# A linear-attention, soft-MoE and feed-forward kernel: the decay tables leave the start of attention, r is scaled out of PSUM, the state's decay goes to GpSimd, half of w1 is loaded in the last chunk

## The chip, the cores and the metric

The kernel runs on one core of a Trainium2 chip. The metric is the device time of one execution in microseconds (us), lower is better. Engines are called as the profile calls them: PE (TensorE; PEld is its weight loads), DVE (VectorE), ACT (ScalarE), POOL (GpSimd), SP (the queue that issues the DMAs here).

## What is computed

Three stages, in float32. First a linear attention with a decaying state, for 4 batches, 8 heads, 768 tokens, head size 48:

```
for t in range(S):
    y[:, :, t] = einsum('bhd,bhde->bhe', r_t, state + outer(u * k_t, v_t))
    state = w * state + outer(k_t, v_t)
```

Its output, 3072 tokens of 384 values, goes through a soft mixture of 8 experts with 4 slots each (logits x @ phi, softmax over tokens and over slots, two matrices w1 and w2 per expert), and then through a feed-forward layer with ELU (w_in 384x2048, w_out 2048x384).

## The kernel before, in words

Attention is done in chunks of 128 tokens: 6 chunks of 4 batches, which are 24 units (un = 4c + b). Inside a chunk the decay is folded into r and k: r is multiplied by powers of w that fall with the token's place, k by powers that grow, so that one matrix product gives all scores of the chunk. Each unit holds 8 heads as 4 pairs, head sizes padded from 48 to 64 (HP), so that a pair fills 128 partitions once it is turned.

**The tables.** DVE builds the powers transposed (head dimension on partitions, token along the row) from L841 to L858: seven squarings, then a doubling of the filled columns, each step waiting for the one ahead; they lie in the buffer of scores. PE turns them into PSUM (L505), DVE multiplies the first r and k out of PSUM (L866), ACT copies the tables to SBUF (L1120) for all later units.

**A unit.** POOL scales r into r_nat (L461), multiplies r by u and by k for the bonus of the diagonal (L466, L468), and scales k into k_nat (L479). PE turns r_nat (turn_r, L512) and k_nat (turn_k, L519); ACT copies the turned r to r_pair (L1100), DVE the turned k to k_pair (L879). PE multiplies the two into the scores in PSUM (attend, L530), adds the old state's part (state_in, L542), turns the former unit's output (turn_x, L569), and multiplies scores with v (values, L561) and k with v (key_values, L552). DVE reduces the bonus (L874), ACT writes the diagonals of the scores (L1106, 8 instructions a unit in two halves), DVE copies the masked scores over them (masked, L884, two a unit), keeps the state (L924 or L926, and the decay L936), and moves the turned output (L890). ACT takes the output out of PSUM (L1111). In each chunk's first two units PE and DVE also make the logits of the chunk ahead (L576, L582, L897 to L903).

**The order** is written out by hand and the same on every engine: in the body of unit un, PE does key_values(un), attend(un+1), state_in(un), turn_x(un-1), turn_r and turn_k(un+2), values(un). DVE does state_sum(un), bonus(un+2), masked(un+1, 0), the decay of un, x_to_sbuf(un-1), masked(un+1, 1), k_to_sbuf(un+2). ACT does y_to_sbuf(un-1), the diagonals of un+1, r_to_sbuf(un+2). The scores have one PSUM buffer, so attend(un+1) waits until both masked copies of un are done (L526). SP loads r and k four units ahead, v three units ahead, and one expert of w1 in every third unit (L351); w2, w_in and w_out follow when their space is free. Most of these last lie over buffers of attention.

After attention (its last values end at 130.8 us) come the expert layers and from about 178 us the feed-forward layer, in which PE is busy throughout.

Of the kernel before, what the change touches and what calls it, by code (L numbers as in the profile page):

```python
# [19 lines left out]
F32 = mybir.dt.float32  # L20
# [6 lines left out]
P = 128  # L27
# [9 lines left out]
def attention_moe_ffn_kernel(nc, r, k, v, w, u, phi, w1, w2, w_in, w_out, out):  # L37
# [22 lines left out]
    with ExitStack() as ctx:  # L60
# [27 lines left out]
        r_raw = place("r_raw", [P, B, H, D], F32)  # L88
        k_raw = place("k_raw", [P, B, H, D], F32)
        u_row = place("u_row", [P, H, D], F32)  # L90
        r_table = place("r_table", [P, H, D], F32)
        k_table = place("k_table", [P, H, D], F32)
        r_nat = place("r_nat", [P, 2, H, HP], F32)
        k_nat = place("k_nat", [P, 2, H, HP], F32)
        assert cursor[0] >= EARLY_AT + 2 * W2_BYTES
# [5 lines left out]
        SCORES_END = cursor[0]  # L101
        y_T = place("y_T", [P, PAIRS, B * P], F32)
        r_pair = place("r_pair", [P, 2, PAIRS, P], F32)
        k_pair = place("k_pair", [P, 2, PAIRS, P], F32)
# [93 lines left out]
        ps_warm = banks[7][:, 0:P]  # L198
# [21 lines left out]
        cleared = sem("cleared")  # L220
        ones_set = sem("ones_set")
        spread_ready = sem("spread_ready")
        powers = sem("powers")
        tables_T = sem("tables_T")
        tables_turned = sem("tables_turned")
        tables_ready = sem("tables_ready")

        r_scaled = sem("r_scaled")
# [80 lines left out]

        PE_TOP_T, PE_TOP_ROWS, PE_SLOT_IN, PE_DEN, PE_SLOT_T = range(1, 6)  # L310
# [23 lines left out]
        def _(sp):  # L334
            def load_rk(c, b):
                tokens = bass.ds(c * P, P)
                sp.dma_start(r_raw[:, b], r_dram[b, tokens]).then_inc(rk_loaded[b], 16)
                sp.dma_start(k_raw[:, b], k_dram[b, tokens]).then_inc(rk_loaded[b], 16)
# [88 lines left out]
        def _(pool):  # L427
# [3 lines left out]
            pool.memset(ones[:, :], 1.0).then_inc(ones_set, 1)  # L431
            pool.memset(ident[:, :], 0.0).then_inc(const_set, 1)
# [15 lines left out]
            pool.memset(r_nat[:, :, :, D:HP], 0.0).then_inc(cleared, 1)  # L448
            pool.memset(k_nat[:, :, :, D:HP], 0.0).then_inc(cleared, 1)
            pool.memset(state[:, :, :, D:HP], 0.0).then_inc(cleared, 1)  # L450
            pool.memset(x_sb[:, :, DM:XW], 1.0).then_inc(cleared, 1)

            def scale_chunk(c, first, last):
                for b in range(B):
                    un, i = c * B + b, b % 2
                    pool.wait_ge(rk_loaded[b], 32 * (c + 1))
                    wait_for(pool, r_turned, un - 1)
                    if first and b == 1:
                        pool.wait_ge(tables_ready, 1)
                    if not (first and b == 0):  # L460
                        pool.tensor_tensor(r_nat[:, i, :, 0:D], r_raw[:, b], r_table[:, :, :],  # L461
                                           ALU.mult).then_inc(r_scaled, 1)
                    pool.wait_ge(r_scaled, un + 1)
                    if first and b == 0:
                        pool.wait_ge(u_loaded, 16)
                    pool.tensor_tensor(r_raw[:, b], r_raw[:, b], u_row[:, :, :], ALU.mult).then_inc(ru_done, 1)  # L466
                    pool.wait_ge(ru_done, un + 1)
                    pool.tensor_tensor(r_raw[:, b], r_raw[:, b], k_raw[:, b], ALU.mult).then_inc(ruk_done, 1)  # L468
                    if first and b == 0:
                        continue  # L470
                    if first and b == 1:
                        pool.wait_ge(tables_ready, 2)
# [796 lines left out]
```

## Time and profile before

| | us |
|---|---|
| median of 3 runs (407.63 to 408.87) | 407.9 |
| the profiled execution, device time | 407.67 |
| its span, first to last instruction | 405.5 |
| PE busy | 384.7 (95%) |
| DVE busy | 275.8 (68%) |
| ACT busy | 219.3 (54%) |
| POOL busy | 114.7 (28%), of it nearly all in attention |
| DMA moved | 51.84 MB |

The profiled execution's own time lies 2.2 us above its span. The busy shares are means over three different stages, so they say little about attention: that has to be read from windows and from the order of time.

### The profile page before, as it was taken

What the parts mean: (1) busy time and instruction counts of PE and PEld (TensorE: products, weight loads), DVE (VectorE), ACT (ScalarE), POOL (GpSimd) and SP (SyncE); (2) the same over time, 40 slices, a digit from 0 to 9 for tenths busy, and PEclk for the clock granted to TensorE, in tenths of its full rate; (3) what the DMA queues carried; (4) which work ended last, traced back from release to release, by engine and by line L of the source; (5) the groups of instructions that cost most, each with busy time, mean ns of one, the idle gap of its engine ahead of it and who ended that gap; (6) DMA issues with size and microseconds to landing.
All of it is one profiled execution on the core that took longest, in us unless ns stands there. A gap on an engine that the chain in (4) does not pass through costs nothing.

```text
span 405.5 us, 9559 instructions
## 1 busy us (share of the span) xinstructions
PE 384.7 (95%) x3528; PEld 341.6 (84%) x3528; DVE 275.8 (68%) x527; ACT 219.3 (54%) x502; POOL 114.7 (28%) x131
## 2 busy tenths in 40 slices
PE   6689999999998799988999999999999999999997
PEld 5588888888886435357999999999999999999996
DVE  4687777877765661079987677677676676776771
ACT  2676757676775214076655544645645465446441
POOL 4998778787870000037410000000000000000000
PEclk8999999999999999999999999999999999999999
DMA  6989899899987879970002000200100020002002
GB/s 128 184 241 259 161 265 267 190 234 270 240 251 290 305 291 423 401 222 18 0 2 78 2 0 2 78 0 0 45 33 0 0 78 0 0 0 78 2 0 78
DMA packets 84802, 51.84 MB, mean 128 GB/s; under 512 B 76704, under 2 KB 81952, under 8 KB 82336
## 3 DMA queue, kind: packets, MB, share of 16 engines
q1 hardware_dynamic: 84768, 51.37, 43.0%
q8 instruction: 23, 0.38, 0.4%
q14 instruction: 11, 0.09, 0.1%
HBM read 45.86 MB, written 4.72 MB: 125 GB/s over the span
## 4 chain that ended last, share of the span: by engine, by line
PE 87%; DVE 5%; issue 3%; POOL 3%; ACT 2%; DMA 0%; SPq 0%; DVEq 0%; POOLq 0%; ACTq 0%
PE psum L823 16%; PE psum L824 16%; PE psum L825 16%; PE psum L530 6%; PE psum L740 5%; PE psum L561 5%; PE psum L569 3%; PE psum L542 3%; PE psum L682 3%; PE psum L663 3%; PE psum L512 2%; PE psum L519 2%; PE psum L552 2%; PE psum L576 2%; PE psum L644 1%
## 5 line engine op out<-in xcount | busy, mean ns | idle before, releaser
L823 PE MATMUL psum<-w_out_hi,elu_hi 128*128 128x384 f32 x372 | 124.8, 336 | 1.3 <-DVE elu_lo L1063 1.3
L824 PE MATMUL psum<-w_out_lo,elu_hi 128*128 128x384 f32 x372 | 125.0, 336 | 0.0
L825 PE MATMUL psum<-w_out_hi,elu_lo 128*128 128x384 f32 x372 | 124.3, 334 | 0.0
L1214 ACT ACTIVATE exp_h<-psum 128x512 f32<-128x512 f32 x95 | 57.1, 601 | 97.3 <-PE psum L740 97.3
L1075 DVE SCALAR_TENSOR_TENSOR elu<-psum,neg_part 128x512 f32<-128x512 f32 x95 | 65.6, 691 | 56.8 <-ACT neg_part L1201 56.8
L824 PEld LDWEIGHTS psum<-w_out_lo,elu_hi 128*128 128x128 f32 x372 | 69.8, 188 | 3.6
L823 PEld LDWEIGHTS psum<-w_out_hi,elu_hi 128*128 128x128 f32 x372 | 69.8, 188 | 2.1 <-DVE elu_lo L1063 2.1
L1063 DVE TENSOR_TENSOR elu_lo<-elu,elu_hi 128x512 fp32r<-128x512 f32 x95 | 69.9, 735 | 0.1
L825 PEld LDWEIGHTS psum<-w_out_hi,elu_lo 128*128 128x128 f32 x372 | 69.9, 188 | 0.0
L1106 ACT ACTIVATE scores<-ident,bonus 128x128 f32<-128x128 f32 x192 | 58.7, 391 | 1.1 <-DVE bonus L874 1.1
L1201 ACT ACTIVATE neg_part<-exp_h 128x512 f32<-128x512 f32 x95 | 59.2, 624 | 0.1
L884 DVE COPY_PREDICATED scores<-mask,psum 128x512 f32<-128x512 uint32 x48 | 35.3, 738 | 13.3 <-ACT scores L1106 11.7
L1088 DVE CAST elu_hi<-elu 128x512 fp32r<-128x512 f32 x95 | 41.5, 437 | 0.1
L740 PE MATMUL psum<-c_T,G_T 128*128 (+1 forms) x95 | 37.1, 392 | 0.1
L487 POOL TENSOR_TENSOR w_out_lo<-w_out_raw,w_out_hi 128x384 fp32r<-128x384 f32 x16 | 17.4, 1107 | 69.5 <-ACT w_out_hi L1183 69.5
L530 PE MATMUL psum<-r_pair,k_pair 64*128 64x128 f32 x384 | 27.9, 284 | 3.6 <-DVE k_pair L879 2.7
L530 PEld LDWEIGHTS psum<-r_pair,k_pair 64*128 64x128 f32 x384 | 23.6, 187 | 5.9 <-issue 3.9
L1111 ACT COPY y_T<-psum 128x512 f32<-128x512 f32 x24 | 14.0, 585 | 23.6 <-PE psum L561 23.6
L561 PE MATMUL psum<-scores,v_sb 128*64 128x128 f32 x384 | 26.3, 279 | 0.0
L466 POOL TENSOR_TENSOR r_raw<-r_raw,u_row 128x384 f32<-128x384 f32 x24 | 24.3, 1012 | 5.6 <-DVE r_nat L866 3.8
L479 POOL TENSOR_TENSOR k_nat<-k_raw,k_table 128x384 f32<-128x384 f32 x23 | 23.1, 1005 | 8.8 <-PE psum L552 8.8
L461 POOL TENSOR_TENSOR r_nat<-r_raw,r_table 128x384 f32<-128x384 f32 x23 | 23.2, 1010 | 5.1 <-DMA k_raw<-in_k_dram 5.1
(145 smaller groups left out, 428.3 us busy)
## 6 DMA issues: line engine op xcount, KB each, us to landing
w_sb<-in_moe_w_dram SPq DMA_DIRECT2D x8, 1536.0 KB, 7.9
w<-in_moe_w_dram SPq DMA_DIRECT2D x8, 1536.0 KB, 8.5
r_raw<-in_r_dram SPq DMA_DIRECT2D x24, 192.0 KB, 4.2
k_raw<-in_k_dram SPq DMA_DIRECT2D x24, 192.0 KB, 4.5
v_sb<-in_v_dram SPq DMA_DIRECT2D x24, 192.0 KB, 4.7
out_dram<-out_sb SPq DMA_DIRECT2D x24, 192.0 KB, 1.9
w_in_sb<-in_moe_w_in_dram SPq DMA_DIRECT2D x3, 1024.0 KB, 13.2
w_out_raw<-in_moe_w_out_dram SPq DMA_DIRECT2D x4, 768.0 KB, 12.2
```

What stands on the lines that cost most here:

```text
L530: m = pe.matmul(ps_A[two][:, a, :], k_pair[rows, i, a, :], r_pair[rows, i, a, :], start=True, stop=True)
L561: m = pe.matmul(ps_y[e0:e0 + HP, two, (a // 2) * P:(a // 2) * P + P], v_sb[:, b, h, :], scores[:, i, h, :], start=(first and a < 2), stop= ...
L740: pe.matmul(banks[4 + f % RING][:, :], G_T[:, f * P:(f + 1) * P], c_T[:, bass.ds(i * BANK, BANK)], start=True, stop=True).then_inc(ffn_don ...
L823: pe.matmul(acc, hi, w_out_hi[:, f, :], start=(f == 0), stop=False)
L824: pe.matmul(acc, hi, w_out_lo[:, f, :], start=False, stop=False)
L825: m = pe.matmul(acc, lo, w_out_hi[:, f, :], start=False, stop=(f == KF2 - 1))
L1063: dve.tensor_tensor(elu_lo[:, f % RING, :], elu[:, f % 2, :], elu_hi[:, f % RING, :].bitcast(F32), ALU.subtract).then_inc(lo_done, 1)
L1075: dve.scalar_tensor_tensor(out=elu[:, f % 2, :], in0=banks[4 + f % RING][:, :], scalar=0.0, in1=neg_part[:, f % 2, :], op0=ALU.max, op1=AL ...
L1088: dve.tensor_copy(elu_hi[:, f % RING, :], elu[:, f % 2, :]).then_inc(hi_done, 1)
L1106: m = act.activation(scores[:, i, h, :], ident[:, :], ACT.Copy, scale=bonus[:, i, h:h + 1])
L1201: act.activation(neg_part[:, f % 2, :], exp_h[:, f % 2, :], ACT.Relu, bias=1.0, scale=-1.0).then_inc(neg_ready, 1)
L1214: act.activation(exp_h[:, f % 2, :], banks[4 + f % RING][:, :], ACT.Exp).then_inc(exp_done, 1)
```

## The change

- The table build alternates squarings and doublings, and the tables stay transposed in an SBUF buffer of their own, tables_T. Only the table of k is turned, for k_nat.
- r is turned as it was loaded (r_raw gets room for the pad) and multiplied by the transposed table when DVE takes it out of PSUM: L879's copy of k becomes a tensor_tensor on r, and the copy of k goes to ACT in the place where r's was. r_nat and POOL's L461 are gone.
- For unit 0 k too is turned as loaded, with 16 small matmuls against the identity, and scaled out of PSUM. Unit 1's k_nat is made by DVE.
- POOL multiplies k_raw in place by u and r; for the first two units it works in r_raw and starts as soon as these are turned. The product state_sum * decay moves from DVE to POOL.
- DVE's bonus reduction moves from the front of a unit's body to its end.
- attend and state_in use 48 rows of each half instead of 64, key_values 48 columns.
- w1: experts 0 to 3 are loaded in units 2, 7, 12 and 17, experts 4 to 7 in the four units of the last chunk. Loads of r and k wait for the turns too; w2_0 and w2_1 have other gates.
- The first matmuls, which keep PE busy, are 6 of 256 columns instead of 8 of 128.

```diff
@@ sync
-                    if un % KD == 1:
-                        load_w1(un // KD)
+                    if last:
+                        load_w1(E // 2 + b)
+                    elif un % 5 == 2:
+                        load_w1(un // 5)
                     if not last:
                         sp.wait_ge(bonus_ready, un + 1)
-                        sp.wait_ge(k_scaled, un + 1)
+                        sp.wait_ge(k_scaled, max(un + 1, 2))
+                        sp.wait_ge(r_turned, un + 1)
+                        sp.wait_ge(k_turned, un + 1)
                         load_rk(c + 1, b)
...
             sp.wait_ge(bonus_ready, UNITS)
+            sp.wait_ge(r_turned, UNITS)
+            load_w2(0)
             sp.wait_ge(kv_done, UNITS - B)
-            sp.wait_ge(r_turned, UNITS)
             sp.wait_ge(k_turned, UNITS)
-            load_w2(0)
+            sp.wait_ge(A_done, UNITS)
             load_w2(1)
@@ gpsimd
+            def k_to_nat(un):
+                pool.wait_ge(rk_loaded[un % B], 32 * (un // B + 1))
+                wait_for(pool, k_turned, un - 1)
+                wait_for(pool, kv_done, min(un - 1, UNITS - B))
+                pool.tensor_tensor(k_nat[:, un % 2, :, 0:D], k_raw[:, un % B], k_table[:, :, :], ALU.mult
+                                   ).then_inc(k_scaled, 1)
+            def products(un):
+                b = un % B
+                pool.wait_ge(k_scaled, un + 1)
+                pool.tensor_tensor(k_raw[:, b], k_raw[:, b], u_row[:, :, :], ALU.mult).then_inc(ru_done, 1)
+                pool.wait_ge(ru_done, un + 1)
+                pool.tensor_tensor(k_raw[:, b], k_raw[:, b], r_raw[:, b, :, 0:D], ALU.mult).then_inc(ruk_done, 1)
+            pool.wait_ge(u_loaded, 16)
+            for un in range(2):
+                pool.wait_ge(r_turned, un + 1)
+                pool.tensor_tensor(r_raw[:, un, :, 0:D], r_raw[:, un, :, 0:D], u_row[:, :, :], ALU.mult).then_inc(ru_done, 1)
+                pool.wait_ge(rk_loaded[un], 32)
+                pool.wait_ge(ru_done, un + 1)
+                pool.tensor_tensor(r_raw[:, un, :, 0:D], r_raw[:, un, :, 0:D], k_raw[:, un], ALU.mult).then_inc(ruk_done, 1)
+            pool.wait_ge(table_ready, 1)
+            pool.wait_ge(k_scaled, 1)
+            k_to_nat(0)
             def scale_chunk(c, first, last):
                 for b in range(B):
+                    un = c * B + b
+                    if un + 2 < UNITS:
+                        k_to_nat(un + 2)
+                        products(un + 2)
+                    if not last:
...
+                        pool.wait_ge(state_summed, un + 1)
+                        if not first:
+                            pool.wait_ge(inter_done, un - B + 1)
+                        pool.tensor_tensor(state[:, b, :, 0:D], state_sum[:, :, :], decay[:, :, :], ALU.mult
+                                           ).then_inc(state_ready, 1)
@@ tensor
-            keep_clock_up(8)
+            for i in (2, 3, 6, 5, 5, 5):
+                pe.matmul(banks[i][:, 0:2 * P].rearrange("p (n t) -> p n t", n=2), ones[:, :],
+                          ones[:, :].unsqueeze(1).broadcast_to([P, 2, P]), start=True, stop=True)
...
+            def turn_k_first():
                 for a in range(PAIRS):
+                    for s in range(2):
+                        for two in range(2):
+                            rows = slice(s * HP, s * HP + HP)
+                            m = pe.matmul(ps_k_first[two * HP:two * HP + D, s, a, :], k_raw[rows, 0, 2 * a + two, :],
+                                          ident[rows, rows], start=True, stop=True, skip_group_check=True)
...
-                        rows = slice(two * HP, two * HP + HP)
+                        rows = slice(two * HP, two * HP + D)
...
-                        m = pe.matmul(ps_kv[two * HP:two * HP + HP, a, :], k_nat[:, i, h, :], v_sb[:, b, h, 0:D],
+                        m = pe.matmul(ps_kv[two * HP:two * HP + D, a, :], k_nat[:, i, h, 0:D], v_sb[:, b, h, 0:D],
...
-            keep_clock_up(1)
-            pe.wait_ge(cleared, 7)
-            turn_r(0, 0)
-            turn_k(0, 0)
-            pe.wait_ge(tables_ready, 2)
+            pe.wait_ge(const_set, 4)
+            pe.wait_ge(pads_set, 1)
+            turn_r(0)
+            turn_k_first()
+            keep_clock_up(2)
+            pe.wait_ge(rk_loaded[1], 32)
+            turn(banks[7], r_raw[:, 1]).then_inc(r_turned, 1)
+            pe.wait_ge(tables_done, 2)
+            for a in range(PAIRS):
+                m = pe.transpose(banks[4][:, a * P:(a + 1) * P], tables_T[:, 1, a, :], ident[:, :])
+            m.then_inc(table_turned, 1)
+            keep_clock_up(2)
             attend(0, 0)
-            turn_r(1, 1)
-            turn_k(1, 1)
+            pe.wait_ge(pads_set, 3)
+            turn_k(1)
@@ vector
+            r_to_sbuf(0, banks[0])
+            dve.wait_ge(k_turned, 1)
+            dve.tensor_tensor(k_pair[:, 0].rearrange("p a (s t) -> p s a t", s=2), ps_k_first,
+                              tables_T[:, 1, :, :].rearrange("p a (s t) -> p s a t", s=2), ALU.mult).then_inc(k_ready, 1)
+            bonus_of(0, r_raw[:, 0, :, 0:D])
+            dve.wait_ge(table_ready, 1)
+            dve.wait_ge(rk_loaded[1], 32)
+            dve.tensor_tensor(k_nat[:, 1, :, 0:D], k_raw[:, 1], k_table[:, :, :], ALU.mult).then_inc(k_scaled, 1)
+            r_to_sbuf(1, banks[7])
             dve.wait_ge(powers, 17)
             dve.tensor_copy(decay[:, :, :], wpow[:, 7, 0, :].unsqueeze(2).broadcast_to([P, PAIRS, D])
...
-                    if not (last and b >= 2):
-                        bonus_of(un + 2, i, (b + 2) % B)
                     if not (last and b == B - 1):
                         masked(un + 1, 1 - i, 0)
-                    if not last:
-                        dve.wait_ge(state_summed, un + 1)
-                        if not first:
-                            dve.wait_ge(inter_done, un - B + 1)
-                        dve.tensor_tensor(state[:, b, :, 0:D], state_sum[:, :, :], decay[:, :, :], ALU.mult
-                                          ).then_inc(state_ready, 1)
...
                     if not (last and b >= 2):
-                        k_to_sbuf(un + 2, i)
+                        r_to_sbuf(un + 2, banks[0])
+                        bonus_of(un + 2, k_raw[:, (un + 2) % B])
@@ scalar
             def attend_chunk(c, first, last):
...
                     if not (last and b >= 2):
-                        r_to_sbuf(un + 2, i)
+                        k_to_sbuf(un + 2)
```

In the changed order ACT does, before the loop: the copy of k's table, the first half of unit 0's diagonals, k_to_sbuf(1), the second half.

## Rows read from the trace of the kernel before

**Rows 1.** Windows: us, busy per engine, PEclk, DMA share, GB/s

```profile
11.60:31.00 19.40, 15.39 (x221) 13.40 (x223) 15.93 (x28) 14.18 (x42) 18.07 (x20) 1.00 0.94 212
50.80:70.00 19.20, 19.16 (x321) 16.82 (x323) 14.74 (x31) 12.91 (x38) 15.77 (x17) 1.00 0.95 267
```

**Rows 2.** Timeline, PE: scores of units 0, 1, 2, 8 (start, us, idle before)

```profile
11.67 1.16 PE L530 MATMUL psum<-r_pair,k_pair 64*128 64x128 f32 x16 [0.88 <-DVE k_pair L879]
16.46 1.16 PE L530 MATMUL psum<-r_pair,k_pair 64*128 64x128 f32 x16 [0.25 <-issue]
21.47 1.16 PE L530 MATMUL psum<-r_pair,k_pair 64*128 64x128 f32 x16 [0.32 <-issue]
...
50.84 1.16 PE L530 MATMUL psum<-r_pair,k_pair 64*128 64x128 f32 x16 [0.78 <-DVE k_pair L879]
```

**Rows 3.** The chain that ended last (start, us): a bonus, and a chunk's logits

```profile
22.12 0.55 DVE bonus L874
...
37.13 1.01 PE psum L576 x32
```

**Rows 4.** The same chain, pieces of a later unit

```profile
66.05 1.09 PE psum L530 x16
67.14 0.60 PE psum L542 x16
...
68.33 0.44 PE psum L512 x4
...
69.20 1.02 PE psum L561 x16
70.22 0.45 PE psum L552 x16
```

**Rows 5.** Timeline, the start

```profile
6.73 0.76 DVE L858 TENSOR_TENSOR scores<-scores,wpow 128x256 f32<-128x256 f32 x2
...
8.70 0.56 DVE L866 TENSOR_TENSOR k_nat<-k_raw,psum 128x384 f32<-128x384 f32 x1
```

**Rows 6.** DMA issues of unit 1's k and of u, with time to landing

```profile
L338 SPq DMA_DIRECT2D k_raw<-in_k_dram x1: 582/582/582, 5.0 to 5.0; - x1
...
DMA to landing us min/median/max: 4.5/4.5/4.5
```

**Rows 7.** Timeline, DVE and ACT in a later unit

```profile
108.50 0.74 DVE L884 COPY_PREDICATED scores<-mask,psum 128x512 f32<-128x512 uint32 x1
109.13 0.67 DVE L879 COPY k_pair<-psum 128x512 f32<-128x512 f32 x1
109.93 0.58 ACT L1111 COPY y_T<-psum 128x512 f32<-128x512 f32 x1 [0.89 <-PE psum L561]
...
110.41 2.45 ACT L1106 ACTIVATE scores<-ident,bonus 128x128 f32<-128x128 f32 x8
```

**Rows 8.** Source lines L936 and L926: ns min/median/max

```profile
L936 DVE TENSOR_TENSOR state<-state_sum,decay x20: 331/344/1011, 19.1 to 112.4; 128x192 f32<-128x192 f32 x20
...
L926 DVE TENSOR_TENSOR state_sum<-state,psum x16: 338/353/355, 34.8 to 110.4; 128x192 f32<-128x192 f32 x16
```

**Rows 9.** Page, costliest groups: POOL's k_nat

```profile
L479 POOL TENSOR_TENSOR k_nat<-k_raw,k_table 128x384 f32<-128x384 f32 x23 | 23.1, 1005 | 8.8 <-PE psum L552 8.8
```

**Rows 10.** Timeline and windows: PE's first matmuls, then the granted clock

```profile
1.70 3.38 PE L496 MATMUL psum<-ones 128*128 128x128 f32 x16 [1.70 <-POOL ones L431]
7.30 1.36 PE L505 MATMUL psum<-ident,scores 128*128 128x128 f32 x8 [2.22 <-DVE scores L858]
...
8.60:9.50 0.90, 0.90 (x6) 0.90 (x5) 0.58 (x2) 0.48 (x1) 0.73 (x1) 0.50 1.14 226
```

**Rows 11.** Weights: DMA rate, first use of w1, wait for w2_7

```profile
128.00:130.00 2.00, 1.48 (x26) 1.14 (x28) 0.23 (x2) 0.46 (x1) 0.00 (x0) 1.00 1.04 432
...
142.37 7.93 PE L663 MATMUL psum<-w_sb,slot_T 128*32 128x512 f32 x72 [0.51 <-DVE slot_T L984]
...
163.31 0.16 PEld L682 LDWEIGHTS psum<-w,hidden_T 128*32 128x32 f32 x8 [0.66 <-DMA w<-in_moe_w_dram]
```

More of the change, by code:

```diff
@@ L101, in attention_moe_ffn_kernel @@
         SCORES_END = cursor[0]
+        tables_T = nc.alloc_sbuf_tensor_at("tables_T", [P, 2, PAIRS, P], F32, offset=cursor[0])
+        cursor[0] += PAIRS * P * 4
         y_T = place("y_T", [P, PAIRS, B * P], F32)
         r_pair = place("r_pair", [P, 2, PAIRS, P], F32)
[L104 removed]
         state = place("state", [P, B, PAIRS, HP], F32)
@@ L463, in scale_chunk @@
[L463 to L472, printed above, removed]
-                        pool.wait_ge(k_scaled, 1)
@@ L474, in scale_chunk @@
-                    wait_for(pool, k_turned, un - 1)
-                    if last and b >= 2:
-                        pool.wait_ge(kv_done, UNITS - B)
-                    else:
-                        wait_for(pool, kv_done, un - 1)
-                    pool.tensor_tensor(k_nat[:, i, :, 0:D], k_raw[:, b], k_table[:, :, :],
-                                       ALU.mult).then_inc(k_scaled, 1)
+                    un = c * B + b
+                    if un + 2 < UNITS:
+                        k_to_nat(un + 2)
+                        products(un + 2)
@@ L482, in _ @@
+                    if not last:
+                        if first and b == 0:
+                            pool.wait_ge(powers, DECAY_SET)
+                        pool.wait_ge(state_summed, un + 1)
[3 more added lines that the diff above has]
+                                           ).then_inc(state_ready, 1)
             attention(scale_chunk)
@@ L539, in state_in @@
                     for two in range(2):
-                        rows = slice(two * HP, two * HP + HP)
+                        rows = slice(two * HP, two * HP + D)
                         e0 = (a % 2) * HP
@@ L605, in attend_chunk @@
                         state_in(un, b, i, c)
+                    if first and b == 1:
+                        pe.wait_ge(r_ready, 2)
                     if not (first and b == 0):
@@ L904, in logits_to_sbuf @@
                                 ).then_inc(logits_ready, 1)
-            k_to_sbuf(0, 0)
-            bonus_of(0, 0, 0)
+            dve.wait_ge(tables_done, 2)
+            r_to_sbuf(0, banks[0])
[7 more added lines that the diff above has]
+            r_to_sbuf(1, banks[7])
             dve.wait_ge(powers, 17)
@@ L910, in _ @@
                             ).then_inc(powers, 1)
-            bonus_of(1, 1, 1)
+            bonus_of(1, r_raw[:, 1, :, 0:D])
             masked(0, 0, 0)
             masked(0, 0, 1)
-            k_to_sbuf(1, 1)
-            dve.wait_ge(powers, 18)
             def attend_chunk(c, first, last):
@@ L1097, in _, with k_to_sbuf @@
         def _(act):
-            def r_to_sbuf(un, i):
-                act.wait_ge(r_turned, un + 1)
-                act.copy(r_pair[:, i], ps_rT).then_inc(r_ready, 1)
+            def k_to_sbuf(un):
+                act.wait_ge(k_turned, un + 1)
+                wait_for(act, A_done, un - 1)
+                act.copy(k_pair[:, un % 2], ps_kT).then_inc(k_ready, 1)
             def diagonals(un, i, two):
@@ L1116, in _ @@
             act.activation(exp_warm[:, :], ident[:, 0:1], ACT.Exp)
-            act.wait_ge(cleared, 7)
-            for n, (table, scaled) in enumerate(((r_table, r_scaled), (k_table, k_scaled))):
-                act.wait_ge(scaled, 1)
-                act.copy(table[:, :, :], banks[2 + n].rearrange("p (h d) -> p h d", h=H)[:, :, 0:D]
-                         ).then_inc(tables_ready, 1)
-                if n == 0:
-                    r_to_sbuf(0, 0)
-            act.wait_ge(tables_turned, 2)
+            act.wait_ge(table_turned, 1)
+            act.copy(k_table[:, :, :], ps_tab[:, :, 0:D]).then_inc(table_ready, 1)
             diagonals(0, 0, 0)
+            k_to_sbuf(1)
             diagonals(0, 0, 1)
-            r_to_sbuf(1, 1)
             def attend_chunk(c, first, last):
```

108 lines of the change are left out of this document (47 added, 61 removed).

## The prediction

> **What bounds the kernel now.** First the windows, to see which engine is full where. From the third chunk on PE is busy 19.16 of 19.20 us, and POOL 15.8: attention there is PE's. In the first chunk POOL is the full one, 18.07 of 19.40 us, PE 15.4 [rows 1]. Then the timeline of PE at each unit's scores, the best clock of progress: units 0, 1, 2 and 8 begin them at 11.67, 16.46, 21.47 and 50.84 [rows 2]. So units 0 to 2 are 4.8 and 5.0 us apart.
>
> What PE itself needs for a unit stands in the chain of waits: 1.09 for the scores, 0.60 for the old state, 0.59 for turning the last output (from 67.74 to 68.33), 0.44 and 0.43 for turning r and k, 1.02 for the values, 0.45 for the new state, together 4.63 [rows 4]. Units of the first chunk have no old state: 4.03. Once a chunk come 1.01 and, with its transpose, some 0.1 for the logits [rows 3]. So the first chunk loses some 0.8 to 1 us a unit to another engine, and later units next to nothing, but that unit 8 waited 0.78 for k_pair [rows 2]. Everything behind attention is untouched and hangs on its end; what can be won lies ahead of unit 8.
>
> **The change, part by part.** I follow the scores of units 0, 1, 2, 5 and 8. A wait costs about 0.1 where a semaphore passes between engines.
>
> *Tables.* Alternating squarings and doublings end no later than the 7.5 us at which they end now [rows 5]; nothing of the new order needs them sooner, as the next item shows. I count this as 0.
>
> *Unit 0.* PE's order puts the turn of unit 1's r, which waits for unit 1's k to land (4.98 + 4.5 = 9.5 [rows 6]), ahead of unit 0's scores. r and k of unit 0, issued first, are there well before; their turning, with 16 small matmuls for k, and two products out of PSUM of about 0.7 each (a 512-column copy is 0.67 [rows 7], 384 columns out of PSUM 0.56 [rows 5]) fill the time up to then and cost nothing while DMA is the later; the cover is about 0.7 us, and beyond it each us is one at unit 0. Then 0.44 for r, 0.44 for the table, 0.44 for two filler matmuls: unit 0's scores begin at 10.9.
>
> *Unit 1.* The table's turn has ended at 10.65, ACT's copy (about 0.5) at 11.2. Now DVE makes unit 1's k_nat, with both inputs in SBUF. Its price is between 0.56, as a product of this size out of PSUM [rows 5], and 1.0: L936, a product of half the size with both inputs in SBUF, takes 0.34 as a rule and up to 1.01 [rows 8], and POOL is busy with products just then. I take 1.0: 12.3. By the Trainium skill, GPSIMD Engine Reference, section 1 (Specifications), POOL shares its SBUF interfaces with DVE and contends with DVE instructions that have two SBUF inputs; the 1.01 agrees, and a sum without that rule would take 0.56 and end 0.45 lower. Then PE turns k (0.1 + 0.66, its pipeline's end counted: 13.05), ACT copies it (0.1 + 0.58: 13.7), and only then makes the second half of unit 0's diagonals (half of 2.45 [rows 7]: 14.95), DVE masks (0.74: 15.7), and unit 1's scores, which wait for that one PSUM buffer, begin at 15.8. That is 0.7 sooner than now. The other arm is shorter: POOL's products and k_nat of unit 0, each 1.005 [rows 9], are done at 13.4 and key_values follows.
>
> *Units 2 to 5.* To unit 2 PE needs 4.03 - 0.59, no output being there to turn: 19.3, now 21.5. POOL per unit drops to k_nat, two products and the decay, of half the size: 3.5 us instead of 4. That is under PE's 4.03, so POOL is no longer the bound, and DVE and ACT are next. bonus_of now stands behind r_to_sbuf, which makes a ring: r_to_sbuf about 0.60 to the next start, bonus 0.55, ACT's diagonals 2.45, masked 0.63 to the next start [rows 3, 7], and 0.2 for two crossings: 4.43. It is over PE's 4.03 in the first chunk. Unit 3 still comes PE's way at 23.4, units 4 and 5 by the ring at 27.8 and 32.2.
>
> *Unit 8.* From unit 4 on PE has state_in too, 4.63 over 4.43, and it is PE's again: three times 4.63 and 1.1 for logits, 47.2. Now it is 50.84 [rows 2]: **3.6 us** won. The 0.78 that unit 8 waits go with it, since POOL's lag behind late loads goes.
>
> *Later units.* The same PE work; r_to_sbuf takes the slot of k_to_sbuf in DVE and the copy of k that of r in ACT. r_to_sbuf reads one operand from PSUM and one from SBUF; L926 does so and takes 0.338 to 0.355 whatever POOL does [rows 8], so I price it as the copy, 0.67 to 0.7. In the last chunk, where PE has no key_values, the later bonus of unit 23 may cost 0.1. The decay on POOL (0.5 by half of 1.005 [rows 9], 1.0 at most) is followed by slack of 1 us a unit, which covers both ends; without it DVE's next state_sum would wait.
>
> *48 rows and columns.* PE's rows know halves of 64 (64x128); nothing shows 48. The time of a matmul follows its columns here: 16 of the scores take 1.09 with 128 columns, and 16 of key_values 0.45 with 48 [rows 4]. I take 0. The other end, two halves no longer side by side, is a rival below.
>
> *w1.* Fewer experts stand in the way of r and k early. In the last chunk four must land: an expert of 1.57 MB takes 3.65 us at 432 GB/s [rows 11], together 14.6. The first is issued about unit 20's scores, near 107 (three chunks of 4 x 4.63 + 1.1 past unit 8's 47.2), the others some 4 us later, and they are first used at 142.4 - 3.5 = 138.9 [rows 11]: more than 10 us of cover. The eight of w2 follow in one queue, and PE already waits 0.66 for the last of them [rows 11]; eleven experts from 111 are 40 us, 151, and the last is wanted at 163.3 - 3.5 = 159.8. So the queue catches up if its gates leave it gaps of no more than 9 us. Cost 0; without that cover each us late would be one us.
>
> **Sum.** 3.6 - 0.1 = 3.5 us from the profiled execution's own 407.67 (its span of 405.5 and 2.2 around it): 404.2. The median of the runs is 407.9, 0.2 above that execution, which I leave inside the range.
>
> **The rivals.**
>
> *The clock is low at the start (0.13): 405.8.* Now PE is busy from 1.70 to 5.08, idle 2.2 us, and then the granted clock is 0.50, 1.2 of 2.4 GHz [rows 10]. After the change PE is idle some 1 to 2 us ahead of unit 1's r. Against it: the first matmuls last longer and the turns follow. If the clock falls for as long as about 3 us while units 0 to 2 begin, PE loses half of that, 1.6 us: 3.5 - 1.6 = 1.9.
>
> *The weights eat it (0.09): 407.2.* Half of w1 lies ahead of w2 in the queue. If the gates leave no gap in which it catches up, w2_7 and w_in stay where they were in time and PE waits the 3 us that attention won. For it speaks the 0.66; against it the 9 us worked out above.
>
> *The ring is slower than PE (0.08): 413.* DVE, ACT, DVE in 4.43 us leave 0.2 a unit to PE's 4.63. If r_to_sbuf is held by POOL as L936 can be (0.67 more [rows 8]), the ring is 5.1: 0.47 over PE in the 13 or so later periods without logits, 6.1 us, and 0.67 in each of 5 early ones, 3.3; against 3.5 won that is 5.9 slower. It decides from r_to_sbuf at 0.9 on, and the kernel is slower than before from about 1.0. Against it speaks L926. By the section of the Trainium skill named above, only two SBUF inputs or a two-port mode contend, and r_to_sbuf has neither; that no run here shows for 512 columns.
>
> *48 rows part the halves (0.05): 423 or more.* Then 16 matmuls at 0.11 each, as a turn over all rows takes (4 in 0.44 [rows 4]), are 1.76 instead of 1.09: 0.67 in 24 units is 16 us, with state_in on top. It may hold for a smaller price.
>
> **Numbers.** My forecast has 0.65. A measurement of this kernel tells about 0.3%, 1.2 us, from no change. Faster: forecast and clock rival but for a little, 0.77. Same: the weights and remnants, 0.10. Slower: ring, rows and a little, 0.13. The range goes from k_nat at its lower end and no new stalls (4.0 won, and 0.6 for what unit 1 may gain when ACT's copy comes sooner): 403.1, up over the clock rival into that of the weights: 407.0.
>
> **What would show it.** Scores of unit 0 near 10.9, unit 1 near 15.8, unit 2 near 19.3, unit 8 near 47.2; from there 4.63 apart. DVE's k_nat near 1.0; r_to_sbuf under 0.75 with POOL busy; POOL under 3.7 us a unit; the matmuls of L530 in 1.09; no wait of the expert stage on w1. I am wrong if units after the eighth are more than 4.7 apart, if the time between attention's end and the feed-forward grows, or if unit 1's scores begin no sooner than 16.5.

## The result, and the profile after

The changed kernel takes 403.63 us (median of 4 runs, 402.58 to 405.00), the kernel before 407.9 (4 runs): a ratio of 0.9893, 95% interval [0.9852, 0.9934]. The forecast was 404.2, range 403.1 to 407.0. The profiled execution took 404.59 of its own, 3.1 less than the one before. Its page:

```profile
span 402.6 us, 9615 instructions
...
PE 386.5 (96%) x3554; PEld 343.9 (85%) x3554; DVE 267.1 (66%) x507; ACT 219.0 (54%) x500; POOL 103.8 (26%) x129
...
PEclk9799999999999999969999999999999999999999
```

PE is busy slightly longer than before, in a shorter span. The third line says why: the granted clock is down in the second slice and again in the eighteenth. The scores of units 0, 1, 2, 3 and 4 in the timeline of PE (start, us, idle before), to be read beside [rows 2]:

```profile
11.01 1.16 PE L561 MATMUL psum<-r_pair,k_pair 48*128 48x128 f32 x16
15.47 2.08 PE L561 MATMUL psum<-r_pair,k_pair 48*128 48x128 f32 x16 [1.26 <-DVE scores L921]
21.90 1.16 PE L561 MATMUL psum<-r_pair,k_pair 48*128 48x128 f32 x16
25.83 1.16 PE L561 MATMUL psum<-r_pair,k_pair 48*128 48x128 f32 x16
30.00 1.16 PE L561 MATMUL psum<-r_pair,k_pair 48*128 48x128 f32 x16 [0.17 <-DVE r_pair L915]
```

Units 0 and 1 stand where they were forecast (10.9 and 15.8). Unit 1's 16 matmuls take 2.08 instead of 1.16, and unit 2 comes at 21.90, not 19.3: later than before the change. Two windows in that stretch give the reason (us, PE busy, PEclk, DMA share, GB/s):

```profile
14.00:15.00 1.00, 0.20 (x10) 0.99 1.42 186
15.00:16.00 1.00, 0.53 (x4) 0.50 1.40 193
...
21.00:22.00 1.00, 1.00 (x22) 0.59 1.45 180
22.00:23.00 1.00, 1.00 (x17) 1.00 1.47 160
```

The clock is at 0.50, 1.2 of 2.4 GHz, for some 6.8 us, where PE has the first chunk's work to do. Before, it was low for 3.4 us around unit 0, of which [rows 10] show a part. Then the lead grows: unit 8 begins at 49.15 against 50.84, 1.7 us ahead, and the last unit at 121.43 against 124.46, 3.0 ahead. From there to the end of the span there are 281.2 us in this profile and 281.0 in that of before: the gain is made inside attention. Behind it two differences cancel. Up to ACT's first write of G_T (171.00, before 174.83) the changed kernel needs 0.8 us less, for PE no longer waits for the last expert of w2 (0.66 in [rows 11]). From there to the end it needs 0.9 more (231.6 against 230.7), and in that stretch its clock is low a second time, from 172 to about 179 us, which it is not in the profile of before:

```profile
172.00:174.00 2.00, 2.00 (x7) 0.50 0.99 307
```

A later unit, in the chain of waits (start, us, what), answers to [rows 4]:

```profile
62.70 1.02 PE psum L593 x16
63.72 0.36 PE psum L584 x16
64.08 1.09 PE psum L561 x16
65.17 0.60 PE psum L573 x16
65.77 0.59 PE psum L601 x4
66.36 0.87 PE psum L530 x8
```

key_values (L584) takes 0.36 where it took 0.45; nothing else moved. The unit is 4.53 us instead of 4.63. The 48 rows of attend and state_in (L561, L573) cost nothing: 1.09 and 0.60 as before.

The start, in the timeline (start, us), down to what releases unit 1's scores:

```profile
9.54 0.66 PE L530 MATMUL psum<-ident,r_raw 128*128 128x128 f32 x4 [1.77 <-DMA k_raw<-in_k_dram]
...
10.67 0.48 ACT L1155 COPY k_table<-psum 128x384 f32<-128x384 f32 x1 [7.86 <-PE psum L626]
...
11.18 0.56 DVE L951 TENSOR_TENSOR k_nat<-k_raw,k_table 128x384 f32<-128x384 f32 x1 [0.37 <-ACT k_table L1155]
11.43 1.18 POOL L486 TENSOR_TENSOR r_raw<-r_raw,k_raw 128x384 f32<-128x384 f32 x1
...
12.79 0.58 ACT L1137 COPY k_pair<-psum 128x512 f32<-128x512 f32 x1 [0.47 <-PE psum L530]
...
13.27 3.61 ACT L1143 ACTIVATE scores<-ident,bonus 128x128 f32<-128x128 f32 x12
...
14.58 0.74 DVE L921 COPY_PREDICATED scores<-mask,psum 128x512 f32<-128x512 uint32 x1 [0.74 <-ACT scores L1143]
```

It is the chain of the forecast link by link: unit 1's k lands, its r is turned, the table is copied, k_nat, the copy of k, the second half of the diagonals, the mask. One link is shorter: DVE's k_nat took 0.56, its lower bound. It began at 11.18, 0.1 us before one of POOL's products ended, and was under way when POOL began the next at 11.43; that one took 1.18 instead of 1.00. The moved operations, by source line (ns min/median/max):

```profile
L503 POOL TENSOR_TENSOR state<-state_sum,decay x20: 592/598/605, 17.5 to 110.7; 128x192 f32<-128x192 f32 x20
L915 DVE TENSOR_TENSOR r_pair<-psum,tables_T x24: 667/674/692, 6.6 to 120.7; 128x512 f32<-128x512 f32 x24
```

### The profile page after: what moved, and what is told of

Same layout as the page of the kernel before. It is cut to its first block, busy times and chain, and to the rows that moved or that the text cites. A ratio compares the mean times of both kernels' runs of the same rounds, so it can differ in the third digit from the quotient of the medians.

```text
span 402.6 us, 9615 instructions
## 1 busy us (share of the span) xinstructions
PE 386.5 (96%) x3554; PEld 343.9 (85%) x3554; DVE 267.1 (66%) x507; ACT 219.0 (54%) x500; POOL 103.8 (26%) x129
## 4 chain that ended last, share of the span: by engine, by line
PE 87%; DVE 4%; ACT 3%; issue 3%; DMA 1%; SPq 1%; ACTq 0%; POOL 0%; DVEq 0%; POOLq 0%
PE psum L865 16%; PE psum L866 16%; PE psum L867 16%; PE psum L561 6%; PE psum L593 5%; PE psum L782 5%; PE psum L530 5%; PE psum L601 3%; PE psum L573 3%; PE psum L705 3%; PE psum L724 3%; PE psum L608 2%; ACT scores L1143 1%; PE psum L584 1%; DMA k_raw<-in_k_dram 1%
## 5 line engine op out<-in xcount | busy, mean ns | idle before, releaser
L1124 DVE CAST elu_hi<-elu 128x512 fp32r<-128x512 f32 x95 | 42.6, 449 | 0.1
L561 PE MATMUL psum<-r_pair,k_pair 48*128 48x128 f32 x384 | 28.8, 291 | 1.9 <-DVE scores L921 1.3
L561 PEld LDWEIGHTS psum<-r_pair,k_pair 48*128 48x128 f32 x384 | 24.1, 193 | 3.9 <-DVE r_pair L915 1.5
L593 PEld LDWEIGHTS psum<-scores,v_sb 128*64 128x64 f32 x384 | 21.2, 140 | 4.2 <-issue 3.5
L1137 ACT COPY k_pair<-psum 128x512 f32<-128x512 f32 x23 | 13.4, 584 | 19.0 <-PE psum L530 19.0
L477 POOL TENSOR_TENSOR k_raw<-k_raw,r_raw 128x384 f32<-128x384 f32 x22 | 22.2, 1007 | 1.7
```

Of the source, the lines that this page charges most:

```text
L561: m = pe.matmul(ps_A[two][:, a, :], k_pair[rows, i, a, :], r_pair[rows, i, a, :], start=True, stop=True)
L593: m = pe.matmul(ps_y[e0:e0 + HP, two, (a // 2) * P:(a // 2) * P + P], v_sb[:, b, h, :], scores[:, i, h, :], start=(first and a < 2), stop= ...
L1124: dve.tensor_copy(elu_hi[:, f % RING, :], elu[:, f % 2, :]).then_inc(hi_done, 1)
```

## The experiments

Single executions of one kernel spread over 3 to 6 us here, more than most parts of the change are worth, so each experiment is read from its trace first and from its median second. "Before" was run beside each of them; its median was 407.89 in the first group (20 runs; the change once more, 64 columns, w1 as before), 407.34 in the second (17; 48 columns alone, ACT's order, fillers, the longer ring) and 407.95 in the third (29; the other four). The changed kernel itself ran only in the first, so an experiment of another group is set against it by their ratios.

**The change once more, for the clock.**

> The changed kernel as it is, for its runs' granted clocks. Theory: its time is 402.6 us where the clock falls once at the start (mean granted clock near 0.996) and about 2.1 us more where it falls twice or for twice as long (near 0.983 to 0.986); runs of one clock agree within 0.3 us. Rival: the spread of 402.6 to 405.0 has nothing to do with the clock, and runs of one clock differ as much.

403.61 us (7 runs, 402.79 to 405.45), ratio 0.9905 [0.9872, 0.9938]. The quickest run had a mean granted clock of 0.996, the slowest two 0.983; but one of 0.992 took 404.52 and one of 0.987 took 403.61. So the clock orders the runs roughly, and something else moves them by 1 us as well: half a hit. The runs of before spread more widely, from 405.8 to 409.8, at clocks from 0.979 to 1.000, and one of 0.996 took 409.44. The profile of this second round has the clock low in the same two places, for 6.8 us from 15.5 and for as long from 172.6.

**64 columns in key_values.**

```diff
-  m = pe.matmul(ps_kv[two * HP:two * HP + D, a, :], k_nat[:, i, h, 0:D], v_sb[:, b, h, 0:D], ...
+  m = pe.matmul(ps_kv[two * HP:two * HP + HP, a, :], k_nat[:, i, h, :], v_sb[:, b, h, 0:D], ...
```

> The changed kernel with key_values at 64 columns again instead of 48; all else stays. Theory (the columns shorten PE's unit): units after the eighth go from 4.53 to 4.62 us apart, attention ends 1.4 to 1.8 us later, key_values' 16 matmuls take 0.45 instead of 0.36. Rival (the 4.53 comes from the new places of the copies, or from 48 rows): 4.53 stays and the time is that of the changed kernel.

404.09 us (6 runs), ratio 0.9918 [0.9883, 0.9953]. The timeline of PE shows it without any doubt:

```profile
62.45 1.16 PE L561 MATMUL psum<-r_pair,k_pair 48*128 48x128 f32 x16
66.52 0.62 PE L584 MATMUL psum<-v_sb,k_nat 128*64 128x48 f32 x16
67.07 1.16 PE L561 MATMUL psum<-r_pair,k_pair 48*128 48x128 f32 x16
```

Units are 4.62 apart again. From unit 5's to unit 23's scores there are 88.5 us (32.16 to 120.70), in the changed kernel 87.1 (34.29 to 121.43): the columns are worth 1.4 us, the lower end of what was expected, and 1.1 of it lies behind unit 8. The units of the first chunk wait for r_pair and those of the last have no key_values. This profile's clock stayed up at the start, so it also shows the forecast of the first chunk undisturbed: units 1, 2, 5 and 8 at 15.99, 19.58, 32.16 and 47.30, where 15.8, 19.3, 32.2 and 47.2 had been worked out. A part of that closeness is luck: unit 0 begins at 11.53 here, 0.6 later than forecast, and counted from it unit 8 comes 0.5 sooner than forecast.

**48 rows and columns alone, in the kernel before.** Two of its first eight filler matmuls go to the bank of key_values, so that its unwritten rows hold numbers.

```diff
-            keep_clock_up(8)
+            keep_clock_up(6)
+            for half in range(2):
+                pe.matmul(banks[6][:, half * P:(half + 1) * P], ones[:, :], ones[:, :], start=True, stop=True)
...
-                        rows = slice(two * HP, two * HP + HP)
+                        rows = slice(two * HP, two * HP + D)
...
-  m = pe.matmul(ps_kv[two * HP:two * HP + HP, a, :], k_nat[:, i, h, :], v_sb[:, b, h, 0:D], ...
+  m = pe.matmul(ps_kv[two * HP:two * HP + D, a, :], k_nat[:, i, h, 0:D], v_sb[:, b, h, 0:D], ...
```

> The kernel before with only 48 columns in key_values and 48 rows in attend and state_in. Theory: units 4.53 apart where PE bounds, some 1.4 to 1.8 us less than before, first chunk as before (unit 2's scores near 21.5). Rival (rows and columns bring nothing): within 0.5 us of before.

The spacing is there:

```profile
65.24 1.16 PE L532 MATMUL psum<-r_pair,k_pair 48*128 48x128 f32 x16
69.77 1.16 PE L532 MATMUL psum<-r_pair,k_pair 48*128 48x128 f32 x16
```

4.53. The time is not: 407.48 (10 runs), ratio 1.0002 [0.9978, 1.0026]. Its profile has the clock low in the second slice and units 1 and 2 at 16.95 and 22.91, later than before, and its runs had mean clocks from 0.971 to 0.992. From unit 8's to unit 23's scores it needs 73.0 us against 73.6, since unit 13 waits 0.50 for k_pair, and behind attention the clock falls once more. So the shorter unit is seen in the trace, 0.6 us of it in these fifteen units, and nothing in the median; the total is inconclusive.

**w1 as before, in the changed kernel.**

```diff
-                    if last:
-                        load_w1(E // 2 + b)
-                    elif un % 5 == 2:
-                        load_w1(un // 5)
+                    if un % KD == 1:
+                        load_w1(un // KD)
```

> The changed kernel with w1 loaded as before, one expert in every third unit from unit 1. Theory (no transfer is waited for after the first chunk in either order): the same within 0.5 us. Rival (moving w1 is what keeps the loads of r and k in time): POOL or PE wait for k_raw around unit 8 again and the time is 0.8 us longer or more.

404.87 us (10 runs, 402.74 to 406.75), ratio 0.9926 [0.9898, 0.9954]: 1.3 over the median of the changed kernel in the same group, but with overlapping runs. The trace sides with the rival. The waits of POOL:

```profile
POOL k_nat L466 <- DMA k_raw<-in_k_dram: 21.6, 8, 4.0
```

POOL waited 21.6 us for k_raw in eight units; in the changed kernel's profile it waited for none. Unit 5 begins 5.55 us behind unit 4 and unit 8 4.89 behind unit 7. From unit 4's scores to unit 23's there are 95.0 us (27.57 to 122.52), in the changed kernel 91.4: 3.5 us lost in this execution, more than the medians say. It was one of the slowest of the ten (406.62), and the quickest, 402.74, can have lost little. My theory was wrong.

**w1 as after, in the kernel before.** The reverse edit.

> The kernel before with only w1 loaded as in the changed one. Theory (experts of w1 ahead of r and k are why POOL waits for k_raw and unit 8 comes 0.78 us late): unit 8's scores near 50.0 and POOL's waits for k_raw under 2 us instead of 5.1, at most 1 us less in all; the expert stage doesn't wait for w1. Rival (those waits are POOL running ahead, or w1's end now comes late): unit 8 as before, or PE waits for w1 behind attention.

407.04 us (8 runs), ratio 0.9967 [0.9936, 0.9998]. POOL's waits for k_raw (5.1 us in six units before) are gone altogether:

```profile
POOL k_nat L481 <- PE psum L554: 12.2, 15, 1.8
POOL r_raw L468 <- DVE r_nat L868: 3.8, 1, 3.8
```

Unit 8 begins at 49.46 instead of 50.84, 0.5 better than expected, though unit 2 begins where it did (21.49 and 21.47). The expert stage begins as soon as its own inputs are there, with no wait for w1. Moving half of w1 is worth about 0.9 us by the medians, barely clear of no change, and 1.4 at unit 8.

**ACT's order in unit 0.**

```diff
             diagonals(0, 0, 0)
-            k_to_sbuf(1)
             diagonals(0, 0, 1)
+            k_to_sbuf(1)
```

> The changed kernel with ACT making both halves of unit 0's diagonals before it copies unit 1's k. Theory (unit 1's scores wait for the copy, then the second half, then the mask): that half starts 0.6 to 0.9 us sooner, unit 1's scores at 14.5 instead of 15.5, unit 2's near 18.4 to 18.6 where the clock stays up, and the whole is 0.7 to 1.0 us less. Rival (unit 1 is held by key_values or by POOL's k_nat): unit 1's scores stay at 15.4.

402.33 us (4 runs, 401.38 to 402.96), ratio 0.9887 [0.9856, 0.9917]. The chain gives way where it was said to (timeline):

```profile
13.01 0.57 ACT L1137 COPY k_pair<-psum 128x512 f32<-128x512 f32 x1
...
14.21 1.16 PE L561 MATMUL psum<-r_pair,k_pair 48*128 48x128 f32 x16 [0.39 <-DVE scores L921]
```

Unit 1's scores follow unit 0's (10.62) by 3.6 us instead of 4.5: 0.9 won. Unit 2 is no test of the rest: it comes at 19.32 and not by 18.6, since the clock is low for 3.4 us ahead of it. In the total the 0.9 isn't proven either, for the interval overlaps that of the changed kernel.

**Fillers in PE's idle places.**

```diff
             turn_k_first()
-            keep_clock_up(2)
+            keep_clock_up(8)
...
             turn_k(1)
+            keep_clock_up(3)
...
                         key_values(un, b, i, c)
+                    if first and b == 0:
+                        keep_clock_up(5)
                     if not (last and b == B - 1):
                         attend(un + 1, 1 - i)
```

> The changed kernel with 14 more filler matmuls in PE's three idle places before unit 1's scores. Theory (the granted clock falls at the start because PE has been idle there): no half clock in the first 25 us in the profile, unit 2's scores near 19.2, and no run's time with the 2 us on top that the fall costs at the start. Rival (the fall is not set by these gaps): it still comes in the profile or the mean clocks of the runs are spread as before.

402.23 us (4 runs, 401.64 to 402.57), ratio 0.9882 [0.9852, 0.9912]. Timeline, then windows (us, busy per engine, PEclk, DMA share, GB/s):

```profile
15.46 1.16 PE L561 MATMUL psum<-r_pair,k_pair 48*128 48x128 f32 x16
18.96 1.16 PE L561 MATMUL psum<-r_pair,k_pair 48*128 48x128 f32 x16
...
12.00:15.00 3.00, 2.78 (x37) 2.45 (x34) 2.26 (x5) 2.53 (x9) 2.20 (x3) 1.00 1.39 181
15.00:18.00 3.00, 3.00 (x37) 2.59 (x37) 1.82 (x5) 2.20 (x8) 2.84 (x4) 1.00 0.46 66
```

The clock stays at 1.00 and unit 2 begins 3.50 behind unit 1, not 6.43. Unit 8 begins at 46.52, 2.6 sooner than in the changed kernel's profile: that is what the low clock cost there. (The profile with 64 columns gives the same from unit 0 to unit 5: 20.6 us where the changed kernel's has 23.3.)

That the fillers kept the clock up is not shown. Three profiles in this document have the changed kernel's start, no fillers, and no low clock there either: 64 columns, w1 as before, and the decay on DVE. With 64 columns PE's idle times before unit 1's scores are 2.3, 0.9 and 1.2 us, no shorter than the 1.8, 0.9 and 1.3 of the changed kernel's profile, where the clock fell. Windows of the decay on DVE and of w1 as before (us, busy per engine, PEclk, DMA share, GB/s):

```profile
14.00:22.00 8.00, 6.58 (x100) 5.89 (x100) 4.99 (x11) 6.58 (x21) 5.22 (x7) 1.00 0.95 152
...
14.00:22.00 8.00, 6.75 (x104) 6.02 (x104) 5.00 (x11) 6.75 (x22) 5.96 (x7) 1.00 0.89 142
```

So the clock falls there in some executions and not in others, and one profile without a fall may be chance. No run of the four went above 402.57, where the changed kernel reached 405.45, but before was quicker in this group too, and by the ratios (0.9882 and 0.9905, intervals overlapping) the fillers may bring 0.9 us or nothing. Two of the four runs still had a mean clock of 0.991, so it falls somewhere in them.

**Both of them,** with only 1 filler instead of 5 ahead of unit 1's scores.

> Both edits that helped: ACT's order of unit 0 and unit 1, and fillers in PE's idle places (10 in all, 1 of them ahead of unit 1's scores). Theory (they add, being two different costs): no half clock in the first 25 us, unit 1's scores at 14.4, unit 2's at 17.9 to 18.3, unit 8's near 45.6, and 0.8 us less than the filler kernel's 402.2. Rival (the first units' own chain takes the place): unit 2's scores at 18.9, the time that of the filler kernel.

402.67 us (6 runs, 400.54 to 404.21), ratio 0.9854 [0.9812, 0.9895]. In the trace they add:

```profile
11.13 1.16 PE L561 MATMUL psum<-r_pair,k_pair 48*128 48x128 f32 x16
...
14.73 1.16 PE L561 MATMUL psum<-r_pair,k_pair 48*128 48x128 f32 x16
...
18.22 1.16 PE L561 MATMUL psum<-r_pair,k_pair 48*128 48x128 f32 x16
```

Unit 8 begins at 45.76, 0.8 ahead of the filler kernel, but the span is 399.4, only 0.3 shorter than its 399.7: behind attention PE's weight load waits 0.75 us for the last expert of w2 (0.52 in the filler kernel, none in the changed one), and the clock is low from 172 for 3.4 us. It has the lowest ratio of all, but its median is not below the other two and its interval overlaps theirs and, by a little, the changed kernel's. It beats the kernel before; whether it beats the changed one or either edit alone the runs don't settle.

**A longer ring.** A copy of 192 columns on DVE ahead of r_to_sbuf, into an unused buffer.

```diff
                 wait_for(dve, inter_done, un - 1 - B)
+                wait_for(dve, idle_done, un - 1)
+                dve.tensor_copy(scratch[:, un % 2, :], turned[:, 0:192]).then_inc(idle_done, 1)
                 dve.tensor_tensor(r_pair[:, un % 2], ...
```

> The changed kernel with a copy of 192 columns, 0.35 us, ahead of r_to_sbuf on DVE in every unit. Theory of the ring (r_to_sbuf, bonus, diagonals, mask, measured 4.29 a unit, PE 4.53): the ring becomes 4.6, units 0.05 to 0.1 further apart, 1 to 3 us in all with 0.35 in each of the first five. Rival (DVE is hidden well below PE): within 0.5 us of the changed kernel.

405.05 us (6 runs, 404.84 to 405.83), ratio 0.9951 [0.9931, 0.9972]: by the ratios 1.9 us over the changed kernel (0.9905 [0.9872, 0.9938]), with intervals that touch. Timeline:

```profile
24.94 1.16 PE L563 MATMUL psum<-r_pair,k_pair 48*128 48x128 f32 x16 [0.36 <-DVE r_pair L919]
29.49 1.16 PE L563 MATMUL psum<-r_pair,k_pair 48*128 48x128 f32 x16 [0.54 <-DVE r_pair L919]
34.04 1.16 PE L563 MATMUL psum<-r_pair,k_pair 48*128 48x128 f32 x16 [0.55 <-DVE r_pair L919]
```

In the first chunk units are 4.55 apart instead of 4.29 and wait for r_pair: the ring is the bound there. Later units stay at 4.53 to 4.55, so PE and the ring are level. From unit 2's scores to unit 23's there are 101.5 us, 1.7 more than in the filler kernel's profile. The reserve of the ring under PE is about 0.25 us a unit, as the forecast had it (0.2).

**The decay back on DVE,** behind the first mask.

```diff
-                        pool.tensor_tensor(state[:, b, :, 0:D], state_sum[:, :, :], decay[:, :, :], ALU.mult
+                        dve.tensor_tensor(state[:, b, :, 0:D], state_sum[:, :, :], decay[:, :, :], ALU.mult
```

> The changed kernel with the product with the decay back on DVE, behind the first mask. Theory (DVE waits for ACT's diagonals there, so it is hidden; POOL is not the bound in either place): where units are 4.53 apart they stay so, and the time is within 0.6 us. Rival (held by POOL up to 1.0 us each it pushes the second mask, r_to_sbuf and the ring): units 0.1 to 0.3 further apart, 2 us or more.

406.11 us (8 runs), ratio 0.9957 [0.9923, 0.9990]: 2.5 over the changed kernel's median and 2.1 by the ratios, whose intervals overlap a little. The rival. Timelines of PE, POOL and DVE:

```profile
24.84 1.16 PE L553 MATMUL psum<-r_pair,k_pair 48*128 48x128 f32 x16 [1.28 <-DVE r_pair L907]
...
51.43 1.01 POOL L477 TENSOR_TENSOR k_raw<-k_raw,r_raw 128x384 f32<-128x384 f32 x1
...
51.51 1.14 DVE L971 TENSOR_TENSOR state<-state_sum,decay 128x192 f32<-128x192 f32 x1
```

The product that takes 0.34 alone ends 0.2 us after POOL's, 1.14 after its start. It pushes x_to_sbuf, the second mask and r_to_sbuf, which stand behind it in DVE's order: the next scores come 5.3 us behind unit 8's (49.12 to 54.38). Units 3, 4 and 5 are late in the same way, unit 3 5.3 us behind unit 2. Together that is 2.8 us from unit 2's to unit 23's scores against the filler kernel's profile (102.7 and 99.9), all of it up to unit 9; behind that units stay 4.53 apart, as the theory had it. Such collisions were there before the change, 0.34 to 1.01 in [rows 8]; that they cost less there because k_to_sbuf was in no ring is argued from the order and was not run.

**Products of units 0 and 1 only after the table.** POOL waits for the first k_nat before it starts on them, and DVE reduces unit 0's bonus after that.

```diff
             pool.wait_ge(u_loaded, 16)
+            pool.wait_ge(k_scaled, 1)
             for un in range(2):
...
-            bonus_of(0, r_raw[:, 0, :, 0:D])
...
             r_to_sbuf(1, banks[7])
+            bonus_of(0, r_raw[:, 0, :, 0:D])
```

> The changed kernel, but POOL starts the products of units 0 and 1 only when the table of k has been applied, and DVE reduces unit 0's bonus after it. Theory (that units 0 and 1 don't wait for the tables is what starts attention early): unit 0's bonus 3.4 us later at about 14, unit 1's scores at 18.5 instead of 15.5, and the whole 3 us longer, so that little of the gain is left. Rival (unit 1 is held by its own k in any case): unit 1's scores by 16.5, less than 1 us longer.

408.4 us (8 runs), ratio 1.0002 [0.9971, 1.0032]: the whole gain is gone. Timeline:

```profile
14.44 0.55 DVE L909 TENSOR_REDUCE bonus<-r_raw 128x8 f32<-128x384 f32 x1 [1.73 <-POOL r_raw L487]
15.02 1.28 ACT L1144 ACTIVATE scores<-ident,bonus 128x128 f32<-128x128 f32 x4 [3.50 <-DVE bonus L909]
...
18.86 1.44 PE L562 MATMUL psum<-r_pair,k_pair 48*128 48x128 f32 x10 [0.46 <-DVE scores L922]
```

Unit 0's bonus is 4.2 us later, unit 1's scores 3.4. The 4.8 over the changed kernel's median is more than these 3.4, and the traces say where the rest lies. Unit 23's scores are 2.5 us later than in the changed kernel's profile (123.90 and 121.43). Another 1.7 stand at the start of the expert stage, where the same 48 matmuls take longer (changed kernel, then this one):

```profile
132.62 4.10 PE L686 MATMUL psum<-x_sb,col_w 128*32 128x386 f32 x48 [1.44 <-ACT col_w L1177]
...
135.09 5.79 PE L687 MATMUL psum<-x_sb,col_w 128*32 128x386 f32 x48 [1.44 <-ACT col_w L1178]
```

The clock is low there from about 135.2 to 138.6. Such a fall, and 1.6 to 1.7 us for it, stand also in the profiles of 48 columns in the kernel before, of w1 as before and of the decay on DVE, so that much of these four spans is the clock's. What brings it about there was not tried. In the profiles, whose clocks are both low for some 7 us at the start, the products' own share is then 2.5 us, near the 3 expected.

## Why the prediction was right

*The bound, and where the gain lies:* right as to place: the gain stands at attention's end and is not given back. That POOL bounds the first chunk rests on the windows; no run relieved POOL alone. The weights did not eat it: PE's wait of 0.66 for the last expert of w2 is gone. But it comes back in three of the four profiles that end attention sooner, 0.34 us with 64 columns, 0.52 with fillers and 0.75 with both edits (with ACT's order alone it doesn't), so that rival stands close behind this change.

*The chain of units 0 and 1:* right in each link. Two runs settle it: with ACT's two links exchanged unit 1 comes 0.9 sooner, with the products held back 3.4 later. The term for DVE's k_nat was mis-sized: taken at 1.0, it was 0.56. The rule of the Trainium skill (GPSIMD Engine Reference, section 1, Specifications), by which POOL and DVE contend when DVE has two SBUF inputs, holds in the trace. In the cases seen the one that began later paid: here POOL, 0.18; in the decay experiment DVE, 0.8. In the experiment on the products, where POOL is idle at that time, DVE's k_nat takes 0.56 as well, so here it paid nothing.

*Units 2 to 5 and the ring:* right in kind. The ring was put at 4.43 and is 4.29 (30.00 to 34.29), since r_to_sbuf takes 0.674 and the crossings less than 0.1 each. Where the clock stayed up, units 2, 5 and 8 came within 0.3 us of the forecast with 64 columns, and 0.3, 0.5 and 0.7 us ahead of it in the filler kernel.

*The ring as the rival that makes the kernel slower:* it did not happen, and the margin was what was said. r_to_sbuf is not held by POOL: 0.667 to 0.692 in 24 executions, one input in PSUM. With 0.35 us more the first chunk's units are paced by it.

*The low clock:* listed at 0.13 and 1.6 us. It did happen in the profiled execution, for 6.8 us instead of 3, and cost 2.6. It must also be set against the kernel before, whose clock falls at the start too. I had taken a full clock as the rule; the runs show it to be one state among several, in both kernels.

*48 columns:* mis-sized. I took 0, with the loss of the paired halves as the only other end. The rows keep their pairs, and the columns are 0.09 us a unit and 1.4 in all. "The time of a matmul follows its columns" was read off the moving columns alone, while the stationary ones count too.

*w1:* the step that failed, though it did not take the time out of the range. "Cost 0" was right for the end of the stream, but the move was given no gain of its own. It has one: 0.9 us by the medians in the kernel before, and 1.3 in the changed one. And it is most of what the prediction put down to POOL between units 2 and 8 ("POOL's lag behind late loads goes"). From unit 2's to unit 8's scores the kernel before needs 29.4 us, with w1 alone moved 28.0, the filler kernel 27.6 (forecast 27.9), and the changed kernel with w1 as before 29.2. So moving w1 is worth 1.4 to 1.6 us there, and all the rest of the change 0.2 to 0.4. In the changed kernel with w1 as before, r and k are asked for later than in the kernel before (unit 5's r at 20.98 instead of 18.40). SP waits there for the bonus, which has moved to the end of the body, but it is also busy longer with the loads ahead; the two were not tried apart.

*The decay on POOL:* costed at nothing, 0.5 with slack behind, and it is 0.598 with slack behind. But what it is worth was missed: it takes a product with two SBUF inputs out of DVE's path to r_to_sbuf, which is in the ring. Left on DVE it would have cost 2.1 us by the ratios and 2.8 in the trace.

So 404.2 was near 403.6 partly by luck, for omissions offset each other. Against the 3.6 us forecast at unit 8, the filler kernel, whose clock stayed up, is 0.7 further ahead there (46.52 against 47.2), and from unit 8 to unit 23 both it and the changed kernel need 72.3 us where the kernel before needs 73.6: another 1.3 won that was forecast as nothing, 1.1 of it the columns. The low clock took 2.6 away: 3.6 + 0.7 + 1.3 - 2.6 = 3.0, the lead at unit 23. The same sum at a full clock is 5.6, and 2.5 of it stand at unit 2.

## What to carry to other kernels

Follow the first units of a pipeline through every engine's order by hand: exchanging two instructions of ACT was worth 0.9 us at unit 1, and nothing in the busy shares points to them. When a step moves from one engine to another, look for rings (an engine that waits for another that waits for the first) and compare the length of each with the bound's: 0.25 us a unit was the whole reserve, and 0.35 more on DVE cost 1.7 us in the trace. When loads are moved about to serve the end of a kernel, price what they free at its start: here that was most of the gain between units 2 and 8. And where single executions differ by more than the effect, the distance of one landmark from the next in the trace still measures a tenth of a microsecond.

## What the runs showed that was not expected

- The stationary operand's columns: 16 matmuls with 48 moving columns take 0.45 us with 64 stationary columns and 0.36 with 48; in the source lines the median instruction falls from 222 to 208 ns.
- Halves with 48 of 64 rows still run side by side: 16 matmuls in 1.09 us either way.
- Idle times of 1.8, 0.9 and 1.3 us in PE's first 15 us were followed by 6.8 us at 1.2 GHz, though PE had worked for 4.35 us from 1.70 on. With 64 columns idle times of 2.3, 0.9 and 1.2 us were followed by none. What decides was not found.
- A second fall, from about 172 to 179 us, stands in the changed kernel's profile and not in that of before, and costs 0.9 us: 231.6 from G_T to the end against 230.7, and 230.7 also in the filler kernel, whose clock stayed up there. A third, near 135 us, stands in four other profiles and costs 1.6 to 1.7 us. What brings them about was not tried.
- DVE's product with two SBUF inputs (0.34 us alone), begun while one of POOL's of 1.00 us was under way, ended 0.2 us after POOL's in the experiment that moved it back: at 23.11, 32.41, 47.38 and 52.65, where POOL's ended at 22.89, 32.20, 47.16 and 52.44.
